# A first slot's tanh taken tile by tile, waits of each exp set per tile, and the split of a last block moved ahead of a leaky step

## The reference

```python
scores = scale * np.matmul(q, k.transpose(0, 1, 3, 2))      # 2 x 12 heads, 448 x 448, head_dim 64
scores = cap * np.tanh(scores / cap)
scores = scores - np.max(scores, axis=-1, keepdims=True)
attn = np.exp(scores)
attn = attn / (np.sum(attn, axis=-1, keepdims=True) + 1e-09)
x = np.matmul(attn, v)                                      # -> 896 tokens x 768
h = x @ w_in;  g = np.where(h > 0.0, h, np.exp(np.minimum(h, 0.0)) - 1.0);  x = g @ w_out
h = x @ w_in2; g = np.maximum(0.01 * h, h);                                 y = g @ w_out2
```

## Time and profile before

| | |
|---|---|
| median of 3 runs | 569.84 us (569.66 to 569.93) |
| the profiled execution, its own time | 571.38 us |
| its span in the profile | 569.6 us |
| PE busy | 558.3 us (98%), 2908 matmuls |
| DVE busy | 467.6 us (82%) |
| ACT busy | 352.7 us (62%) |
| POOL busy | 285.8 us (50%) |
| the chain that ended last, by engine | PE 89%, DVE 5%, ACT 3%, issue 2% |
| PE's waits for ACT's tanh (L1113 <- L619) | 2.1 us in 3 |
| PE's waits for DVE's low parts (L1128 <- L792) | 2.1 us in 4 |
| a load of k, issue to landing (median) | 3.1 us |
| a load of a weight unit | 384.0 KB, 3.1 us to landing (median) |

### The profile page before, as it was taken

The page is one execution under the profiler, slowest core; times in us unless marked ns, Lnnn a source line. Parts: engine busy times, 40 slices in busy tenths (PEclk is TensorE's granted clock), DMA queues, the critical chain, the costliest instruction groups (busy, mean ns, idle before and its releaser), DMA issues.

```text
span 569.6 us, 8610 instructions
## 1 busy us (share of the span) xinstructions
PE 558.3 (98%) x2908; PEld 503.2 (88%) x2908; DVE 467.6 (82%) x754; ACT 352.7 (62%) x606; POOL 285.8 (50%) x277
## 2 busy tenths in 40 slices
PE   7999999999999999999999999999999999999997
PEld 6777789889998999999999999999999989899996
DVE  4899998878875233898989999989999789999871
ACT  5999998999996355654644455546454445544440
POOL 5879999799975755552000008967576520000000
PEclk8999999999999999999999999999999999999999
DMA  6466665455423233335644422031123226436351
GB/s 174 95 163 140 150 147 145 123 141 138 99 64 91 84 118 109 113 92 167 217 135 151 149 89 83 1 111 56 57 62 105 63 78 226 139 110 218 85 173 49
DMA packets 34172, 67.07 MB, mean 118 GB/s; under 512 B 6864, under 2 KB 18768, under 8 KB 34128
## 3 DMA queue, kind: packets, MB, share of 16 engines
q1 hardware_dynamic: 33984, 66.28, 40.5%
q10 hardware_dynamic: 144, 0.23, 0.1%
HBM read 63.70 MB, written 2.80 MB: 117 GB/s over the span
## 4 chain that ended last, share of the span: by engine, by line
PE 89%; DVE 5%; ACT 3%; issue 2%; POOL 0%; ACTq 0%; POOLq 0%
PE mlp_ps L1154 9%; PE mlp_ps L1156 9%; PE mlp_ps L1155 9%; PE o_ps L1154 6%; PE o_ps L1156 6%; PE o_ps L1155 6%; PE scores L1154 5%; PE scores L1156 5%; PE scores L1155 5%; PE probs_t L1128 5%; PE probs_t L1155 4%; PE probs_t L1156 4%; PE probs_t L1154 4%; PE scores L1113 3%; PE scores L1114 3%
## 5 line engine op out<-in xcount | busy, mean ns | idle before, releaser
L562 POOL TENSOR_TENSOR w_lo<-w_raw,w_hi 128x768 fp32r<-128x768 f32 (+1 forms) x62 | 103.1, 1665 | 57.3 <-ACT w_hi L649 56.8
L649 ACT ACTIVATE w_hi<-s_sum 128x768 fp32r<-128x768 f32 (+1 forms) x64 | 43.7, 685 | 80.9 <-DVE s_sum L908 54.2
L649 ACT ACTIVATE w_hi<-w_raw 128x768 fp32r<-128x768 f32 (+1 forms) x77 | 56.5, 737 | 31.6 <-PE o_ps L1156 16.0
L629 ACT ACTIVATE soft<-soft,neg_max 112x448 f32<-112x448 f32 x96 | 64.0, 683 | 0.2 <-DVE soft L785 0.2
L785 DVE TENSOR_SCALAR_CACHE_REDUCE soft<-soft,neg_abs 112x448 f32<-112x448 f32 x96 | 60.8, 670 | 2.8 <-ACT soft L619 2.5
L562 POOL TENSOR_TENSOR w_lo<-s_sum,w_hi 128x384 fp32r<-128x384 f32 x32 | 42.2, 1330 | 23.0 <-ACT w_hi L649 23.0
L1154 PE MATMUL mlp_ps<-x_hi,w_hi 128*128 128x448 f32 x132 | 49.2, 373 | 0.0
L792 DVE TENSOR_TENSOR p_lo<-probs_t,p_hi 112x896 fp32r<-112x896 f32 x37 | 40.3, 1090 | 10.7 <-ACT p_hi L638 10.6
L1156 PE MATMUL mlp_ps<-x_hi,w_lo 128*128 128x448 f32 x132 | 48.3, 366 | 0.0
L1155 PE MATMUL mlp_ps<-x_lo,w_hi 128*128 128x448 f32 x132 | 48.3, 366 | 0.0
L619 ACT ACTIVATE soft<-scores 112x896 f32<-112x896 f32 x47 | 43.9, 935 | 6.6 <-PE scores L1114 6.6
(11 more groups left out here) (241 smaller groups left out, 1765.9 us busy)
## 6 DMA issues: line engine op xcount, KB each, us to landing
w_raw<-w_units SPq DMA_DIRECT2D x120, 384.0 KB, 3.1
q_raw<-qT SPq DMA_DIRECT2D x24, 224.0 KB, 3.2
k_raw<-kT SPq DMA_DIRECT2D x23, 224.0 KB, 3.1
v_raw<-v_rows SPq DMA_DIRECT2D x24, 112.0 KB, 3.8
inv_all<-inv_rows SPq DMA_DIRECT2D x24, 112.0 KB, 3.0
y_t<-y_out SPq DMA_DIRECT2D x12, 224.0 KB, 2.8
inv_rows<-row_inv SPq DMA_DIRECT2D x24, 1.8 KB, 2.8
k_raw<-kT ACTq DMA_DIRECT2D x1, 224.0 KB, 3.3
```

The costliest lines, as they stand in the source:

```text
L562: pool.tensor_tensor(w_part(w_lo, n), w_source(n), f32(w_part(w_hi, n)), ALU.subtract).then_inc(w_lo_pool, 1)
L629: nc.scalar.activation(soft[0:QT, b, t, :], soft[0:QT, b, t, :], ACT.Exp, bias=neg_max[:, c, t:t + 1], scale=-1.0, accum_out=row_sum[:, h ...
L649: nc.scalar.activation(w_part(w_hi, n), w_source(n), ACT.Copy).then_inc(w_hi_done, 1)
```

## The change

1. A semaphore is given by `score(0)` after its first tile. `tanh(0)` becomes two instructions, one a tile, whose scale is read from `s_scale` in memory, one value a partition; the first waits for the first tile alone. The load of `scale_reg` moves behind `tanh(0)`.
2. `maxima(0)` waits for each tile's tanh by itself, and `split_k0(1)` moves behind `maxima(0)` in DVE's program.
3. `exp(k)` waits for each tile's maxima by itself, in all 48 slots.
4. Behind the loop over the blocks, ACT runs `g_high(1, 2)` ahead of `leak(7, "p4")`, and DVE runs `g_low(1, 2)` ahead of `block_hidden(7, "p4")`. The differences of row 7, which DVE made ahead of that step, now come behind it.

```diff
--- before.py
+++ after.py
@@ -296,6 +296,7 @@
         q_loaded, k_loaded, v_loaded = ([sem(f"{n}_loaded{i}") for i in range(2)] for n in "qkv")
         w_loaded = [sem(f"w_loaded{i}") for i in range(RAW)]
         y_stored = sem("y_stored")
+        first_scores, first_tanh = sem("first_scores"), sem("first_tanh")
         zero_set, ident_set, ident_ready = sem("zero_set"), sem("ident_set"), sem("ident_ready")
         cap_step, cap_ready = sem("cap_step"), sem("cap_ready")
         k0_hi_done, k0_split = sem("k0_hi_done"), sem("k0_split")
@@ -613,6 +614,15 @@
             scale_reg = act.alloc_register("scale_reg")

             def tanh(k):
+                if k == 0:
+
+                    act.wait_ge(first_scores, 1)
+                    nc.scalar.activation(soft[0:QT, 0, 0, :], scores[0:QT, 0, 0:SEQ], ACT.Tanh, scale=s_scale[0:QT, 0:1]
+                                         ).then_inc(first_tanh, 1)
+                    act.wait_ge(scores_done, 1)
+                    nc.scalar.activation(soft[0:QT, 0, 1, :], scores[0:QT, 1, 0:SEQ], ACT.Tanh, scale=s_scale[0:QT, 0:1]
+                                         ).then_inc(tanh_done, 1)
+                    return
                 act.wait_ge(scores_done, k + 1)
                 if k >= SOFT:
                     act.wait_ge(transposed, k - SOFT + 1)
@@ -622,10 +632,10 @@
             def exp(k):
                 h, half = divmod(k, 2)
                 b, c = k % SOFT, k % 2
-                act.wait_ge(neg_max_done, 2 * k + 2)
                 if half == 0 and h >= 2:
                     act.wait_ge(den_done, h - 1)
                 for t in range(2):
+                    act.wait_ge(neg_max_done, 2 * k + t + 1)
                     nc.scalar.activation(soft[0:QT, b, t, :], soft[0:QT, b, t, :], ACT.Exp, bias=neg_max[:, c, t:t + 1],
                                          scale=-1.0, accum_out=row_sum[:, h % 2, 2 * half + t:2 * half + t + 1]
                                          ).then_inc(exp_done, 1)
@@ -722,8 +732,9 @@
                 cols = slice(part * SEQ // 2, (part + 1) * SEQ // 2)
                 nc.scalar.activation(q_stack[:, 0, cols], q_raw[:, 0, cols], ACT.Copy).then_inc(q0_hi_done, 1)
             act.wait_ge(cap_ready, 1)
-            act.reg_load(scale_reg, s_scale[0:1, 0:1].bitcast(mybir.dt.int32))
             for s in range(STEPS):
+                if s == 1:
+                    act.reg_load(scale_reg, s_scale[0:1, 0:1].bitcast(mybir.dt.int32))
                 if s < SLOTS:
                     tanh(s)
                 if 1 <= s <= SLOTS:
@@ -771,8 +782,8 @@
                     w_high(GEMM2[1] + (q - GEMM2[1] + 6) // 2)
                 if q in (GEMM2[1] - 4, GEMM2[1] - 2):
                     g_high(1, (q - GEMM2[1] + 4) // 2)
+            g_high(1, 2)
             leak(HF - 1, "p4")
-            g_high(1, 2)
             second(1)

         @block.vector
@@ -780,8 +791,11 @@
             def maxima(k):

                 b, c = k % SOFT, k % 2
-                dve.wait_ge(tanh_done, k + 1)
+                if k:
+                    dve.wait_ge(tanh_done, k + 1)
                 for t in range(2):
+                    if k == 0:
+                        dve.wait_ge(*((first_tanh, 1), (tanh_done, 1))[t])
                     nc.vector.tensor_scalar(soft[0:QT, b, t, :], soft[0:QT, b, t, :], neg_abs[0:QT, 0:1], BIG, ALU.mult,
                                             ALU.min, accum_out=neg_max[:, c, t:t + 1]).then_inc(neg_max_done, 1)

@@ -1007,10 +1021,11 @@
             nc.vector.reciprocal(cap_inv[:, :], cap_abs[:, :]).then_inc(cap_step, 1)
             dve.wait_ge(cap_step, 4)
             nc.vector.tensor_scalar(s_scale[:, :], cap_inv[:, :], float(HD) ** -0.5, None, ALU.mult).then_inc(cap_ready, 1)
-            split_k0(1)
             for s in range(STEPS):
                 if s < SLOTS:
                     maxima(s)
+                if s == 0:
+                    split_k0(1)
                 for u in units_ending_at(s - 1):
                     hidden(u)
                 if 2 <= s <= SLOTS + 1:
@@ -1075,15 +1090,17 @@
                     c = ("p1", "p5", "p3").index(p)
                     first_difference(1, c)
                     third_difference(1, c)
-                if i >= 3 and p == "p4":
+                if 3 <= i < HF - 1 and p == "p4":
                     first_difference(1, i)
                     third_difference(1, i)
                 if q + 8 < GEMM2[1] and q + 8 >= GEMM1 + 14 and q + 8 in SUM_ITEMS:
                     weight_sum(q + 8)
                 if q in (GEMM2[1] - 4, GEMM2[1] - 2):
                     g_low(1, (q - GEMM2[1] + 4) // 2)
+            g_low(1, 2)
             block_hidden(HF - 1, "p4")
-            g_low(1, 2)
+            first_difference(1, HF - 1)
+            third_difference(1, HF - 1)
             second(1)
             dve.wait_ge(u3_done, 2 * HC)
             for t in range(HC):
@@ -1112,6 +1129,8 @@
                     rows = slice((2 * half + t) * QT, (2 * half + t + 1) * QT)
                     nc.tensor.matmul(dst[0:QT, t, 0:SEQ], q_stack[:, b, rows], k_hi[:, b, :], start=True, stop=False)
                     last = nc.tensor.matmul(dst[0:QT, t, 0:SEQ], q_stack[:, b, rows], k_lo[:, b, :], start=False, stop=True)
+                    if k == 0 and t == 0:
+                        last.then_inc(first_scores, 1)
                 last.then_inc(scores_done, 1)

             def transposes(k):
```

## The result

Median after 571.93 us (569.46 to 574.49, 12 runs), before 570.28 us (569.18 to 571.28, 12 runs beside them): ratio 1.0035, 95% interval 1.0022 to 1.0048. I had forecast 569.4 (568.7 to 570.4) and gave "slower" 0.04. The median lies outside the range.

What follows compares the result with a forecast made beforehand. PE was taken to bound the kernel (busy 98%), with ACT pacing the first 80 us. 0.3 us at the start plus 0.1 in the last block, off 569.84, gave 569.4 us; range 568.7 to 570.4.

Steps and rivals of the forecast that it cites:

- the second head's k split, moved behind the maxima: DVE at the start: split runs 8.80 to 9.85 us, so score(2) starts at 9.95, 0.77 later than before.
- with POOL in the way: Bound on the moved k split: POOL adds up to 0.33 us, score(2) at 10.28 and tanh(2) at 11.35.
- rival (d): Start: PE idles 1.45 us, score(2) runs at 1.2 GHz, tanh(3) at 14.74; 570.1 us, or 570.45 with POOL; chance 0.12.
- won 0.3 us: Start: tanh(3) comes at 13.95 to 14.1 us instead of 14.35; bounds 0.08 and 0.65 us won.
- The tanh of one tile: ACT, slot 0: tanh(0) of 0.92 us becomes two instructions of 0.67 us each, ending at 7.34 and 8.09.
- The register load: ACT, between tanh(0) and tanh(1): takes 0 to 0.9 us, taken as hidden; up to 0.46 us delay otherwise.
- `exp(0)`: ACT, slot 0: follows tanh(1) at 9.46 us at the latest instead of 9.70, 0.24 us won.
- The waits of the exps: 48 more waits on ACT, all already met: cost 0, from above 0.2 us; nothing to win either.
- Item 2's stall: Last block: PE's 0.43 us loss at item 2 goes, as g_low(1, 2) ends at 467.63 us.
- 0.1 us kept: Last block: of the 0.43 us only the 0.1 us by which DVE's chain moves is kept; bounds 0 and 0.5.
- a wait of 0.5 at item 5: Last block: loads delay the sum for item 6 and g_low(1, 5), so PE waits 0.5 us at item 5.
- a sign of being wrong: Last block: the forecast is wrong if item 5 starts as soon as PE is ready.

Runs made afterwards that it cites:

- e3: Changed kernel with 16 unread transposes on PE between score(1) and score(2) to fill PE's pause: 570.72 us, ratio 1.0016 to the kernel before.
- e5: The changed kernel again, unedited, one profiled execution: 571.65 us (span 569.9, clock 0.997).
- e5b: The changed kernel again, with only a blank line added, one profiled execution: 569.5 us (span 567.7, clock 0.997).
- e9a: The changed kernel again, one execution to catch a long one in a profile: 573.15 us (span 571.4, clock 0.997).
- e4: Kernel before with only split_k0(1) moved behind maxima(0): 572.85 us, ratio 1.0038 to the kernel before.
- e9b: The changed kernel again, one execution to catch a long one in a profile: 573.23 us (span 571.4, clock 0.994).
- e6: Changed kernel with POOL's third-head split held back until DVE's split_k0(1) is done: 569.75 us against 569.42 before, ratio 1.0010.
- e1: Changed kernel with split_k0(1) back in its old place ahead of maxima(0): 568.92 us against 570.25 before, ratio 0.9982.
- e8: Changed kernel with split_k0(1) back in its old place, and score(2) also waiting for slot 1's first maximum: 569.67 us against 569.73 before, ratio 1.0003.
- e2: Kernel before with only the last block's new order (part 4 of the change): 569.22 us, ratio 0.9995 to the kernel before.
- e7: Kernel before with only each exp's wait for its own maxima in all slots (part 3): 569.9 us against 569.42 before, ratio 0.9999.
- e10: Kernel before with tanh(0) by tiles, the moved register load and first maxima by tile, without the moved split: 569.96 us against 569.73, ratio 0.9996.

## Why the prediction was wrong

**The step that failed** is the second head's k split, moved behind the maxima, and in it the price of POOL at work beside it: "starts at 8.80 and ends at 9.85", with POOL in the way "up to 0.33 more", which is an end at 10.18 and `score(2)` at 10.28. It ends at 9.88 to 10.08 in the short executions and at 11.92 and 13.04 in the two long ones that were profiled, up to 3.2 us late. I had taken the upper bound from one pair of rows, of an instruction that overlapped POOL by chance, and had looked at POOL's row at 7.94 only for its end. Behind it POOL works without a hole until 12.33 us. The split was moved into this stretch. That the short execution has `score(2)` at 9.93 and `tanh(3)` at 13.95, as forecast, is luck: the split started 0.36 us sooner than I had it (8.44) and took 0.39 more (1.44 for 1.05), and the two errors cancel.

What the price depends on can be read from the eight profiles with the moved split. Ends are start plus duration:

```
        CAST          ends 0.24-0.26 after      k_lo ends   0.46-0.49 after POOL's
e3      8.62 -  9.08  POOL's  8.84 (first)       9.98        9.51
after   8.44 -  8.98          8.73 (first)       9.88        9.40
e5      8.56 -  9.20          8.95 (first)      10.08        9.62
e5b     8.42 -  9.10          8.84 (first)       9.99        9.51
e9a     8.33 -  9.94          9.69 (second)     11.92       11.45
e4      9.50 - 11.14         10.89 (second)     12.61       12.12
e9b     8.45 - 11.57         11.32 (fourth)     13.04       12.56
e6      8.67 -  9.25          9.01 (first)       9.92        none (0.63 alone)
```

In brackets: whether that was the first POOL instruction that ran beside the cast, the second or the fourth. Each of the two DVE instructions ends a fixed time after the end of some POOL instruction, but for the second one of e6, beside which POOL stood still. It seems to wait until POOL lets go, and where POOL's next instruction gets in first, it waits for that one too; where DVE gets in first, POOL's next is the one that is stretched (0.70 and 0.92 us for 0.56 in after). So the price is not a slower rate but a number of lost turns, of 0.56 to 1.12 us each: none in the short executions (there each waits for one POOL instruction to end and for no other), one in e4, three in e9b, two in e9a (one at the cast, one at the subtraction, which passed L526's end at 10.35 and ended behind L529's). The Trainium skill, SBUF — State Buffer, Who interferes with whom, says that of a VectorE instruction in a 2-port mode, or one with two SBUF inputs against a GpSimd one that reads SBUF, and a GpSimd instruction, whoever issues first gets the shared pair for the whole instruction and the other is blocked. The traces agree that one waits until the other has ended; but by that rule one would expect the wait to be for one POOL instruction, at most 1.1 us here, and the cast of e9b waited for four. That this is what holds the split up is read from the ends in the table; no run shows the port itself.

That the overlap with POOL makes the long executions is shown: e6 takes away most of it by one wait, and of its 12 runs none is over 571, nor any of the 23 runs of e1 and e8, which have the split in its old place, against 8 of 16 executions of after (12 and the four again). What decides who gets the next turn is not. In e9a and e9b POOL's q landed later than in after (its L526 at 7.38 and 7.40 instead of 6.95), so that L532 still had 0.8 and 0.7 us to go when the cast started, against 0.3; but in e4 it was L525 with 0.3 us to go, and the turn was lost as well.

**The second cause: the clock**, rival (d), to which I gave 0.12. "Against: it fell only at 11.3" was read off one execution; it fell at about 9.8 in e5, 11.0 in e8 and 12.0 in e9b. The pause that I had at 1.45 us was 2.25 in after, since PE was done with `score(1)` sooner. With PE idle for 1.7 to 2.6 us before `score(2)` a stretch at 1.2 GHz follows in half of the runs or more (e6 8 of 12, e8 7 of 12), with 4.3 to 5.6 us it was there in all three profiles, and of the 77 runs of before, with a pause of 0.68 us in the one that was profiled, 9 have a clock of 0.997 or less. What one such stretch costs depends on where it lies: 0.98 us at `tanh(3)` in e5 (14.93 - 13.95, 0.2 of it from a later split), 0.41 in before, nothing in e5b. I had priced it at 0.7 over the forecast and that was about right; but I had POOL's part in it at 0.33 more, where it was up to 3. For a long execution the two add: e9b is 4.0 us behind the short one at `tanh(3)`, of which 13.09 - 9.93 = 3.16 is the later `score(2)` and the rest the clock. Six executions of 12 being 2 to 5 us longer than the others lifts the median by the 1.65 that was measured. It lies in the gap between the groups, between spans of 569.1 and 571.2, and one run more or less in either group would move it by about a microsecond.

**The baseline was one execution too.** Its own time was 571.38 us, 1.5 over the median of 569.84. The 14.35 from which I won 0.3 us contained 0.41 us for a stretch at 1.2 GHz; without it that head would have had `tanh(3)` at 11.03 + 2.91 = 13.94. So after's 13.95, which I forecast almost exactly, is no gain, and against the execution of e2, whose `score(0)` was as fast as after's or faster, it is a loss of 13.95 - 13.57 = 0.4 us even when all goes well. Only its 77 runs show that before mostly runs at clock 1.000. The forecast also said that `score(0)` ran at 1.2 GHz in before. Its matmuls were as slow as those in the stretch at 0.50 (0.58 us), but the granted clock of the windows from 2 to 8 us reads 1.00 there, so no row shows it. The 1.87 us that rival (d) took from it came out even so (12.02 - 10.14 = 1.88 in e5, at 0.50).

**What held.** The tanh of one tile: 0.64 and 0.62 against 0.67. The register load: hidden. `exp(0)`: not later than 9.46, and e1, whose PE starts as slowly as that of before, shows the 0.24 as 0.35. The waits of the exps: nothing over 23 slots, though in slot 0 they do win where the scores are there early (e7 against e2, with `tanh(1)` at 7.91 and 7.88: 0.46 us at `tanh(3)`), which I had ruled out. Item 2's stall went. Of the last block I had 0.1 us kept, because of a wait of 0.5 at item 5, and had called it a sign of being wrong if item 5 started as soon as PE was ready. It nearly does: the step from item 4 to 5 is 3.70 in after and 3.81 to 3.96 in the other executions with the new order, against 3.64 to 3.78 without it and 3.65 with no wait at all. The loads did come sooner (0.38 us of waiting for 0.83), which I had argued against. From the start of item 0 to that of item 7 it is 25.8 to 26.15 us in ten executions with the new order and 26.07 to 26.4 in four without it, so some 0.3 is kept on average. e2 shows no gain beyond the noise, as 0.3 us of 570 wouldn't.

**A version that beats both**: e1, the whole change without the moved split, 0.18% below before (0.10 to 0.27%). It keeps the early `exp(0)` (tanh by tiles), PE's short pause of 0.73 us, and with it the clock in all 11 runs. How much of the 1.3 us is its own is not shown. The profiles account for about 0.35 at the head and 0.3 in the last product, and its shortest span is 566.8 against 567.1 in the 31 runs of before beside it. The rest may be the two paces of the last product (below): seven of its 11 spans are at 567.2 or less, against three of those 31, and the other two batches of before have medians 0.5 and 0.8 us lower.

## What to carry to other kernels

A VectorE instruction that is moved into a stretch where GpSimd works without a hole isn't priced by its duration alone: list GpSimd's instructions there, and reckon that the moved one may have to wait for several of them, not for one. Before a baseline is taken from a profile, look at its granted clock in the stretch that matters, since a gain over a slow stretch of the baseline is none. And when the median moves by more than any mechanism of the profiled execution explains, look at all spans with their clocks: two groups mean that the profile shows one of them.

## What the runs showed of the hardware that I had not expected

- A cast of 128x448 that takes 0.38 us alone took 0.46 to 3.12 beside GpSimd's splits, and the subtraction behind it 0.85 to 1.95 instead of 0.63, in steps given by the ends of GpSimd's instructions.
- From about item 8 of the last product on, the items of one execution take either 3.65 or 3.72 us each (the same 18 matmuls, granted clock 1.000 in both). Before, after, e3, e5, e7 and e10 were profiled with 3.72, e1, e2, e4, e5b, e6, e8 and e9b with 3.65, and e9a went from 3.65 to 3.72 at item 13. From item 8 to the end that is 1.2 us (those at 3.65 have one step of 3.84 at item 12), as much as most effects here, and it fits the gap that the spans of e10 show (five from 567.0 to 567.1, seven from 568.0 to 568.6). It took a part in neither cause: e9b is long with 3.65. What decides it stays open.
- The stretch at 1.2 GHz differs in length: in e9b it lasted from about 12 to past 18 us, in before from 11.3 to 14.7, in e5 from about 9.8 to 13.2.
